# Scatters of the third group moved three blocks later, and three more expert chunks split behind the FFN

## What is computed

```python
# 1 linear attention: B=2, H=8, S=768, D=48  ->  x: 1536 rows x 384
# 2 FFN with a leaky gate:
h = x @ w_in                       # 384 -> 2048
g = np.maximum(h, 0) + alpha * np.minimum(h, 0)
x = g @ w_out                      # 2048 -> 384
# 3 mixture of 8 experts, one expert for each row:
logits = x @ w_gate
expert_idx = np.argmax(logits, axis=1)
# gate_w: softmax probability of the chosen expert
disp[e, counts[e]] = x[i]          # rows placed in their expert's table, at most 384 each
h = np.maximum(disp @ w1[e], 0)    # 384 -> 1024
y = h @ w2[e]                      # 1024 -> 384
out[i] = gate_w[i] * y[expert_idx[i], pos[i]]
```

## Time and profile before

| what | value |
|---|---|
| median of 3 runs | 448.55 us (447.76 to 449.93) |
| profiled execution, its own time | 447.43 us |
| span in its profile | 445.5 us |
| mean granted TensorE clock | 0.991 |
| FFN and routing inside it, without the last routing | about 60 to 270 us of the span |
| last routing, up to the first expert product | 270 to 289 us |
| experts | 289 to 440 us |

### The profile page before, as it was taken

How to read it: one execution, slowest core, us unless ns; L and a number is a source line. 1 busy time by engine, 2 the same in 40 slices (tenths; PEclk the granted TensorE clock), 3 DMA queues, 4 the chain that set the end, 5 groups by cost and what they waited for, 6 DMA issues and landing times.

```text
span 445.5 us, 9385 instructions
## 1 busy us (share of the span) xinstructions
PE 420.5 (94%) x3333; PEld 406.7 (91%) x3333; DVE 257.6 (58%) x555; ACT 197.1 (44%) x450; POOL 176.3 (40%) x189
## 2 busy tenths in 40 slices
PE   5799999999999999999999986799999999998893
PEld 5688889999999999999999985699999999998893
DVE  6898867675435333643438564444668584648820
ACT  2799943432311123111223432244568674558731
POOL 3999725553323523244436860520110310012112
PEclk9999999999999999999999999999999999999997
DMA  7995034427960100000012440495676866563000
GB/s 248 403 355 188 3 113 147 151 89 253 371 220 14 40 1 0 0 23 31 0 35 71 142 147 15 141 346 191 185 235 190 258 193 204 159 214 107 10 19 7
DMA packets 33935, 61.45 MB, mean 138 GB/s; under 512 B 4654, under 2 KB 26910, under 8 KB 33888
## 3 DMA queue, kind: packets, MB, share of 16 engines
q1 hardware_dynamic: 31008, 55.53, 38.5%
q0 software_dynamic: 2880, 5.29, 3.5%
HBM read 47.53 MB, written 14.79 MB: 140 GB/s over the span
## 4 chain that ended last, share of the span: by engine, by line
PE 80%; DVE 7%; ACT 5%; issue 3%; POOL 2%; DMA 0%; POOLq 0%; DVEq 0%; ACTq 0%
PE bank L1152 20%; PE bank L1167 20%; PE bank L1277 17%; PE bank L1306 14%; ACT scores L613 3%; PE bank L1055 2%; PE bank L1264 1%; PE bank L1121 1%; ACT w_high L596 1%; DVE scores L828 1%; DVE neg L886 1%; PE bank L1085 1%; DVE act_full L892 1%; PE bank L1113 1%; PE bank L1176 1%
## 5 line engine op out<-in xcount | busy, mean ns | idle before, releaser
L512 POOL TENSOR_TENSOR g_low<-act_full,g_high 128x384 fp32r<-128x384 f32 x63 | 63.6, 1010 | 114.6 <-ACT g_high L642 114.6
L642 ACT ACTIVATE g_high<-act_full 128x384 fp32r<-128x384 f32 x64 | 33.7, 526 | 149.9 <-DVE act_full L892 137.3
L1152 PE MATMUL bank<-x_split,w_high 128*128 (+1 forms) x384 | 98.3, 337 | 0.0
L886 DVE TENSOR_SCALAR neg<-bank,alpha_sb 128x384 f32<-128x384 f32 x64 | 39.2, 613 | 71.5 <-PE bank L1152 71.4
L568 POOL DMA_INDIRECT out<-y_out,token x24 | 25.1, 1046 | 122.3 <-ACT y_out L729 121.0
L1152 PEld LDWEIGHTS bank<-x_split,w_high 128*128 128x128 f32 x384 | 69.0, 188 | 0.2 <-issue 0.2
L1167 PE MATMUL bank<-w_high,g_high 128*128 128x384 f32 x189 | 65.1, 344 | 1.1 <-POOL g_low L512 1.1
L1152 PE MATMUL bank<-x_split,w_low 128*128 (+1 forms) x192 | 64.4, 336 | 0.0
L1167 PE MATMUL bank<-w_high,g_low 128*128 128x384 f32 x189 | 63.8, 337 | 0.0
L1167 PE MATMUL bank<-w_low,g_high 128*128 128x384 f32 x189 | 63.7, 337 | 0.0
L1277 PE MATMUL bank<-xe_high,w_high 128*128 128x256 f32 (+1 forms) x192 | 58.0, 302 | 1.8 <-DVE xe_low L1005 1.8
(11 more groups left out here) (127 smaller groups left out, 794.2 us busy)
## 6 DMA issues: line engine op xcount, KB each, us to landing
w_raw<-chunks SPq DMA_DIRECT2D x96, 192.0 KB, 3.1
w_raw<-chunks SPq DMA_DIRECT2D x32, 384.0 KB, 3.2
rk_in<-att_rk SPq DMA_DIRECT2D x12, 704.0 KB, 6.1
routed_rows<-fill SPq DMA_DIRECT2D x1, 5211.0 KB, 16.8
xe<-routed_rows SPq DMA_DIRECT2D x7, 579.0 KB, 5.5
v_in<-att_v SPq DMA_DIRECT2D x12, 200.0 KB, 6.1
out<-fill SPq DMA_DIRECT2D x1, 2304.0 KB, 23.4
x_split<-x_split POOLq DMA_DIRECT2D x18, 48.0 KB, 2.7
```

The costliest lines, as they stand in the source:

```text
L512: pool.tensor_tensor(gl[:, f % 4, :], act_full[:, f % 2, :], gh[:, f % 4, :].bitcast(f32), ALU.subtract).then_inc(s_gl, 1)
L642: act.activation(gh[:, f % 4, :], act_full[:, f % 2, :], ACT.Copy).then_inc(s_gh, 1)
L886: dve.tensor_scalar(neg[:, f % 2, :], h, 0.0, alpha_sb[:, f:f + 1], ALU.min, ALU.mult)\
L1152: last = mm(bank[f % 4][:, 0:G], a[:, f, w], x[:, kc, bass.ds(g * G, G)], start=kc == 0 and i == 0, stop=kc == KC - 1 and i == 2)
```

## The change

`DEFER` goes from 2 to 5, so the last group's blocks split chunks 16 to 22, and chunks 23 to 31 are split behind the FFN. The scatters of a group run in blocks 12 to 14 of the next group in place of blocks 9 to 11, for all three groups that have a next one. Behind the FFN POOL splits chunks 23 to 25 ahead of the last scatters, the others behind them. ACT splits 23 to 25 ahead of the register loads, 26 and 27 behind them and ahead of `xe_high`; DVE splits 23 to 27 behind its register loads and ahead of `xe_low`. SP issues no chunk load between its loop (up to chunk 27) and the wait for the scatters; chunks 28 to 31 all follow the landing of expert 0's rows.

```diff
-    DEFER = 2
+    DEFER = 5
 # SP
-            for m in range(DEFER):
-                load_chunk(2 * NF - RAW + m, m)
             sp.wait_ge(s_scat, 16 * T)
...
-            for m in range(DEFER, RAW):
+            for m in range(RAW):
                 load_chunk(2 * NF - RAW + m, m)
             load_xe(1)
 # POOL, in the groups 1 and 2, and the same in the last group
-                    if 9 <= f < 9 + GT:
-                        scatter(g - 1, (f - 9,))
+                    if 12 <= f < 12 + GT:
+                        scatter(g - 1, (f - 12,))
 # POOL, behind the FFN
             rows_there(NG - 2)
+            for c in range(2 * NF - 4 - DEFER, 2 * NF - 6):
+                split_low(c)
             scatter(NG - 1)
...
-            for c in range(2 * NF - 4 - DEFER, 2 * NF):
+            for c in range(2 * NF - 6, 2 * NF):
                 split_low(c)
 # ACT
-            for c in range(2 * NF - 4 - DEFER, 2 * NF - 4):
+            for c in range(2 * NF - 4 - DEFER, 2 * NF - 6):
                 split_high(c)
             act.wait_ge(s_cnti, 1)
             rows = [rows_of(act, e) for e in range(E)]
-            split_high(2 * NF - 4)
+            for c in range(2 * NF - 6, 2 * NF - 4):
+                split_high(c)
             for i in range(GT):
                 xe_high(0, i, bank[4 + i])
-            for c in range(2 * NF - 3, 2 * NF):
+            for c in range(2 * NF - 4, 2 * NF):
                 split_high(c)
 # DVE
-            for c in range(2 * NF - 4 - DEFER, 2 * NF - 3):
+            for c in range(2 * NF - 4 - DEFER, 2 * NF - 4):
                 split_low(c)
             for i in range(GT):
                 xe_low(0, i, bank[4 + i])
             keep_meta(0)
-            for c in range(2 * NF - 3, 2 * NF):
+            for c in range(2 * NF - 4, 2 * NF):
                 split_low(c)
```

More of the change, by code:

```diff
@@ L554, in _ @@
                     g_low(NG - 1, f)
-                if 9 <= f < 9 + GT:
-                    scatter(NG - 2, (f - 9,))
+                if 12 <= f < 12 + GT:
+                    scatter(NG - 2, (f - 12,))
                 if 4 <= f < NF - DEFER:
```

## The result

| | before | after |
|---|---|---|
| median, runs | 448.74 us, 6 runs (447.24 to 449.99) | 452.45 us, 6 runs (452.10 to 453.69) |
| profiled execution, its own time | 447.43 us | 453.64 us |
| its span | 445.5 us | 451.7 us |
| its mean granted clock | 0.991 | 0.974 |

The ratio is 1.0079, with a 95% interval from 1.0059 to 1.0099: slower by 3.7 us in the medians, where 3.8 were forecast. The two profiled executions differ by more, 6.2 us, so the difference of the traces has to be taken apart before it is read. Two marks that the change doesn't touch serve for that: the first FFN product (59.29 in the trace of before) and the first expert product (289.06).

The account below looks back on a forecast made before the run. PE bounds the kernel, waiting only at the FFN's end and in the last routing. SP's issue of expert 0's rows +1.25 - 1.3 + 2.2, together 2.2, plus 0.5 and 1.1: 3.8 on 448.55, so 452.3 us; 8-in-10 range 449.4 to 454.6.

Parts of the forecast that it names:

- Part 1: End of the FFN: without splits of chunks 23 to 25 DVE keeps up, PE's wait at block 14 goes, 1.3 us gained.
- Part 2: Blocks 12 to 14: the moved scatters fit on POOL and land before `x2` is copied; cost nothing.
- Part 3: Last routing: POOL's three low parts ahead of the last scatters hold up DVE's places; slots and count 2.2 us late.
- Part 4: Behind the last routing: chunk 27's load waits for DVE; expert 0's rows issued 2.2 us late, plus 0.5 for transfer.
- Part 5: Expert 0's ups: chunks 28 and 29 ahead of expert 1's rows make PE wait 1.1 us (bounds 0 and 1.5).
- (c): Expert 0's first products: clock falls after PE idles, half speed up to 3 us, loses 1.5; 453.5 us; chance 0.10.
- (a): Last routing: DVE slips between POOL's low parts, hold 0 to 0.5 us; time about 449.7; chance 0.18.
- (b): Last routing: FFN gain goes through, count and chunk 27's load early; gain at most 0.1, 448.3 us; chance 0.06.
- (d): End of the FFN: DVE isn't unblocked, the stall at 267.14 stays; 1.3 us more, 453.6; chance 0.04.

Follow-up runs that it names:

- e1: Kernel before with only the scatters moved, from blocks 9 to 11 to blocks 12 to 14, chunks 16 to 25 still split in the blocks; 449.11 us, ratio 1.0000.
- e11: Kernel before with only the scatters moved, to blocks 11 to 13, no split deferred; 447.90 us, ratio 0.9970.
- e2: Changed kernel with the scatters back in blocks 9 to 11; 452.13 us, ratio 1.0081 to the kernel before.
- e3: Changed kernel with POOL's low parts of chunks 23 to 25 behind the last scatters; 452.74 us, ratio 1.0102 to the kernel before.
- e12: Changed kernel, chunks 23 to 25: DVE's low parts ahead of its register loads, POOL's behind the last scatters; 450.04 us, ratio 1.0038 to the kernel before.
- e4: Changed kernel with DVE's low parts of chunks 23 to 25 ahead of its register loads; 451.22 us, ratio 1.0050 to the kernel before.
- e9: Changed kernel with 9 of its 24 dummy transposes moved from ahead of expert 0's transposes to behind them; 451.96 us, ratio 1.0058 to the kernel before.
- e5: Changed kernel with 9 more dummy transposes ahead of the transposes of expert 0's rows and 9 behind; 456.60 us, ratio 1.0173 to the kernel before.
- e10: e7 with chunk 31's high part on ACT and low part on DVE behind expert 0's ups; 447.49 us, ratio 0.9975 to the kernel before.
- e6: Kernel before with 9 more dummy transposes between expert 0's transposes and its first product; 450.44 us, ratio 1.0038.
- e8: e7 with the 9 dummy transposes of e6; 450.63 us, ratio 1.0048 to the kernel before.
- e7: Kernel before, only chunk 25 moved behind the FFN, chunk 28 loaded before the scatter wait, expert 1's rows ahead of chunks 29 to 31; 448.49 us, ratio 0.9987.

## Why the prediction was right

**Part 1, right.** The down of block 14 starts without a wait. From the first FFN product to the `logits` of the last group it is 213.17 us before (272.46) and 211.87 after (272.56 in its trace): 1.30 us gained, 1.3 forecast. What the prediction left out is why DVE was late. It named the chain to ACT's weight copies; e1 and e11 show that the scatters' place had nearly as large a part (1.05 of the 1.30 us in e1), since they made POOL late and so caused the 1.82 us of the earlier trace rows. The trace of e2 has no wait there either: each half of the change removes most or all of it by itself.

**Part 2, right as a cost, with less room than forecast.** e2, with the scatters back in their blocks, takes 452.13 to the changed kernel's 452.45. But in e1, where the splits still delay block 14, the same scatters are late and hold up `x2` by 1.17 us. With the split gone POOL reaches the scatter of block 14 in time, but only just: it starts at 265.79, `rows_there` ends at 269.1, and `x2` is copied at 269.69. The prediction had the landing 2.5 to 3 us behind the start and 1.3 us to spare; it took 3.3, and 3.85 in e1, and 0.6 were left.

**Part 3, right.** Three operations of DVE were each held through one of POOL's. From the start of `lsh` (the subtraction that opens `choose` behind the maximum) to that of the count it is 2.76 us before (274.24 to 277.00) and 4.78 after (274.33 to 279.11): 2.0 us, 2.2 forecast. The rule of the Trainium skill that I weighed there would have had 2.8, with `row` and `slot_i` held as well; they started as the streak ended (`row` at 278.43, POOL's third part to 278.48), and were not. Its section "Who interferes with whom" on the same page says that whoever issues first has the ports for the whole instruction. The trace agrees for the copies, which got in between two of POOL's operations; the large low parts of e3 and e12 waited through a whole streak, so behind which of several queued POOL operations DVE comes is not told by the rule, and differed here.

**Part 4, right, sizes a little high.** SP's issue of expert 0's rows, counted from the first FFN product, is at 223.26 us before (282.55) and 225.17 after (285.86): 1.9 late, where 2.2 were forecast; the register loads took 5.26 us, not 5.67. Landing is 2.50 late (290.71 to 286.81, less 1.40), 2.7 forecast, so chunk 27 in front of the rows cost 0.6, as against 0.5. The first expert product is 2.29 late, 2.7 forecast: from the landing to it took 2.04 us, not 2.25. e4 and e12 change this order and that of part 3, and take 1.9 us away mark to mark and 2.4 in the medians, while the scatter held by DVE gives 0.9 back.

**Part 5, right in kind, its size open, and covered in the profile by rival (c).** With the clock at 1.00 the wait for expert 1's rows is 1.15 us in e9 and 1.87 in e5, 1.1 forecast with 1.5 as upper bound. In the profiled execution it is nothing, because the clock fell as rival (c) had it, to 0.81 and 0.62, and cost 2.53 us, where (c) had put 1.5. The prediction added wait and clock as separate cases; they are in place of each other. The median loss, 3.7 us, is 2.3 to the first expert product (from one trace of each) and, by subtraction, 1.4 behind it, forecast 2.7 and 1.1. That 3.8 met 3.7 this closely is in part luck: the two errors are opposite, and the second share is not shown to be the wait of part 5. It may as well be a net of executions with slow and with fast first products on both sides: e1, whose time is that of the kernel before, had 7.92 us for its four ups in its profile. How often each kernel has slow first products was not measured.

**Rivals.** (a) and (b) needed a hold of DVE near zero and an early load of chunk 27; both fell with the trace. (b)'s gain does exist where nothing stands in front of scatters and rows: e10 and e11. (d) fell with part 1.

## What to carry to other kernels

Work that is moved out of a full loop into a serial stretch is not free there, even on an idle engine: ask which queue it stands in front of (here SP waited for a split behind eight register loads), whether it holds up the engine on the path (here POOL's low parts held DVE), and what its later loads push back. When PE waits at the end of a loop for an engine that is behind, look first at what made that engine late; moving each group's three scatters by two blocks gave 0.9 us mark to mark (e11), most of the 1.3 that deferring three more chunks gained at that place, and cost nothing. Compare profiles from mark to mark: 1.4 of the 6.2 us between these two lay ahead of the change.

## What the hardware showed that I had not expected

- A large DVE subtraction with both operands in SBUF waited for a streak of POOL subtractions to end, not for the one in progress: 1.82 us behind two (before), 2.92 and 2.96 behind the rest of four (e3, e12), 0.56 alone. Each ended 0.42 to 0.43 us behind POOL's last. Copies and scalar operations of 3 elements a partition got in after one (0.82 to 0.84 us, after). What makes the difference, the size or the kind of operation, is open.
- It works the other way round as well: an indirect DMA on POOL took 1.93 us in place of 0.99 while DVE subtracted (e4), and 1.91 in e12.
- Granted clock from 293 to 300 us, in expert 0's first ups, was 1.00 in nine of the profiled executions and 0.62 to 0.86 in five (after, e1 to e4), and for two of them the work just ahead doesn't tell why: e1 and the kernel before had nearly the same idle time ahead of the first product (1.62 and 1.77 us); PE was busy 4.24 of 6 us from 283 to 289 in the trace of before, 5.47 of 6 in e1, and it was e1's that fell (0.81, then 0.86).
- Nine more dummy transposes on PE cost 1.7 to 2.1 us in the medians (e6 against before, e8 against e7) at an unchanged mark to mark, in e6 with a wait of 2.66 us "issue" some 120 us later. The cause is open.
